# Rows for the first two expert tiles gathered from a copy of x in DRAM, with tokens found by one-hot products

## The chip, the cores and the metric

The kernel runs on one core of a Trainium2 chip. The metric is the device time of one execution in microseconds (us), the median over the runs shown. PE is TensorE, ACT is ScalarE, DVE is VectorE, POOL is GpSimd and SP is SyncE.

## What is computed

Three stages run in one program: causal-by-block attention (4 batches, 8 heads, 576 positions, head width 64), a mixture of 8 experts with hidden width 1024, of which each token takes one or none, and a dense two-layer network of hidden width 2048. The part around the change:

```python
x = attn_out.transpose(0, 2, 1, 3).reshape(2304, 512)
do_compute = (x @ w_skip) > 0            # the others pass through
logits = x[do_compute] @ w_gate
e_idx = argmax(logits, axis=1)           # one of 8 experts
gate_w = softmax(logits)[e_idx]
for e in range(8):
    h = relu(x[e_idx == e] @ w1[e])
    y[e_idx == e] = gate_w * (h @ w2[e])
x = x + y
# then: h = x @ w_in; out = (max(h,0) + alpha*min(h,0)) @ w_out
```

## The kernel before

**Attention** works on 16 pairs of heads (four pairs to a batch). SP's queue feeds it with one `load_step(n)` for each pair: it waits for `split_done` (POOL has split the queries and keys of the next pair into high and low parts), issues six loads of q and k for pair n+2 (lines 364 and 367), the two copies of `q_t` for the first head of pair n+1 (`swap`, line 388, which waits for ACT's evacuations `qk_evac`), three loads of v, the other two copies, and 512 KB of zeros into `x_slots`. In pairs 1 to 8 the queue also issues 1 MB of expert weights in each pair (lines 426 and 428). All of SP's DMAs go in one queue in this order. PE's first scores of pair n+1 wait for the first head's two copies (`swapped[0]`). The results for tokens land in `x_tok` (128 tokens of a tile on the partitions, 18 tiles, 512 columns), and the last 64 tokens of each batch first in `x_tail`, which ACT copies into the last two tiles of `x_tok` when attention is over.

**Routing** is a chain of small operations on DVE, with PE's products `RANKS` and `COUNTS` in the middle. It ends with `slot_i` (line 1192): for each token, the row of `x_slots` at which it is to stand, so that the tokens of an expert fill whole tiles of 128 rows. The semaphore `routed` goes out with it. POOL then issues 18 indirect DMAs (line 555), one for each tile of `x_tok`, which scatter the tokens' rows into `x_slots` in DRAM; SP meanwhile writes 15 tiles of zeros into the unused part of `y_slots` (line 454). When all 18 scatters have landed SP loads the rows of expert tile 0, and when these have landed those of tile 1 (`load_rows`).

**An expert tile** takes 128 rows: ACT copies them from `rows_in` to `rows`, PE transposes them (line 773), DVE takes them out as `rows_t`, PE multiplies by `w1` (line 786, 64 matmuls), ACT and DVE make `h_hi` and `h_lo`, and PE multiplies by `w2` in three products (line 800, 24 instructions to a tile). There are 13 such tiles here: expert 0 has tile 0, expert 1 tile 1, and expert 2 tiles 2 and 3. Each `w2` is needed as high and low parts. For experts 0 and 1 ACT and DVE make them (lines 966 and 1229 the first halves, 972 and 1240 the second). From expert 2 on POOL makes the first halves (lines 575 and 578), and PE waits for them in `w2_split` ahead of line 800.

**POOL's order** is: the 18 scatters, a wait for both row loads (`rows_loaded`, line 559), two chunks of `w_in` of 1 MB each (`stage`, loaded at line 564 and split at 566 and 568, with one buffer for both), the first halves of `w2` for experts 2 to 7, and then the gathers and splits of the dense network.

## Time and profile before

| | |
|---|---|
| time, median of 3 runs | 910.12 us (907.75 to 910.98) |
| time of the profiled execution | 910.3 us |
| span from first to last instruction | 908.4 us |
| PE busy | 822.5 us, 91% of the span |
| DVE / ACT / POOL busy | 435.7 / 265.2 / 238.0 us |
| mean granted TensorE clock | 0.960 of full speed |

The profiled execution is within 0.2 us of the median, and 1.9 us of it lie outside the span. Attention ends at about 246 us, routing at 256.5 us, the first matmul of an expert tile starts at 288.95 us, and the dense network's first matmul at 484.77 us. Times in the rows below are microseconds from the start of the span.

### The profile page before, as it was taken

How to read it: one execution, taken by the hardware profiler on the slowest of the kernel's cores; microseconds unless marked ns; L12 is line 12 of the kernel's file. 1: busy time of each engine (PE TensorE's matmuls, PEld its weight loads, DVE VectorE, ACT ScalarE, POOL GpSimd, SP SyncE). 2: the span in 40 equal slices, each digit the busy share in tenths (PEclk: the TensorE clock that was granted, in tenths of full speed). 3: DMA queues.
4: the chain of work that ended last, by engine and by line, in shares of the span. 5: the costliest groups of instructions: out<-in, count | busy, mean ns of one | idle time of the engine just before them, and what ended most of it. 6: DMA issues, size and time to landing. Idle time of an engine off the chain costs nothing.

```text
span 908.4 us, 15588 instructions
## 1 busy us (share of the span) xinstructions
PE 822.5 (91%) x5243; PEld 724.0 (80%) x5244; DVE 435.7 (48%) x894; ACT 265.2 (29%) x643; POOL 238.0 (26%) x193
## 2 busy tenths in 40 slices
PE   6799999999703989999968999999999999999997
PEld 5588888888503979999857988998998998898986
DVE  3476776777741333323364554444354344443442
ACT  4466656656321212212311112112112112112111
POOL 6224244432053681230547861001001001000000
PEclk9899999999955999999997999999999999999999
DMA  6388888574166846613834312002002002000001
GB/s 127 75 237 211 228 230 207 145 174 112 37 228 236 301 185 208 229 48 127 311 141 116 91 35 70 0 0 69 0 0 69 0 0 69 0 0 35 1 1 35
DMA packets 95972, 99.66 MB, mean 110 GB/s; under 512 B 64336, under 2 KB 64336, under 8 KB 95440
## 3 DMA queue, kind: packets, MB, share of 16 engines
q1 hardware_dynamic: 87136, 70.79, 27.3%
q0 software_dynamic: 4448, 15.73, 5.5%
q10 hardware_dynamic: 4368, 12.88, 3.9%
q8 instruction: 11, 0.18, 0.1%
q14 instruction: 9, 0.07, 0.0%
HBM read 64.78 MB, written 24.12 MB: 98 GB/s over the span
## 4 chain that ended last, share of the span: by engine, by line
PE 75%; SPq 6%; POOL 5%; DMA 5%; issue 4%; DVE 3%; ACT 2%; DVEq 0%; ACTq 0%; POOLq 0%
PE bank L836 22%; PE bank L847 22%; PE bank L786 7%; PE bank L800 7%; PE bank L685 4%; PE bank L696 3%; PE bank L673 3%; POOL x_slots L555 2%; PE bank L719 2%; PE bank L649 2%; SPq L364 2%; PE bank L667 1%; SPq L388 1%; DMA stage<-in_moe_w_in_dram 1%; POOL wi_lo L568 1%
## 5 line engine op out<-in xcount | busy, mean ns | idle before, releaser
L1287 DVE TENSOR_SCALAR g_sb<-bank,alpha_sb 128x384 f32<-128x384 f32 x96 | 59.3, 618 | 218.8 <-PE bank L836 218.6
L1005 ACT CAST g_hi<-g_sb 128x384 fp32r<-128x384 f32 x96 | 49.4, 515 | 322.0 <-DVE g_sb L1289 322.0
L836 PE MATMUL bank<-u_hi,wi_hi 128*128 128x384 f32 x384 | 130.5, 340 | 1.4 <-DVE u_lo L1260 1.4
L836 PE MATMUL bank<-u_hi,wi_lo 128*128 128x384 f32 x384 | 130.4, 340 | 0.0
L836 PE MATMUL bank<-u_lo,wi_hi 128*128 128x384 f32 x384 | 130.0, 339 | 0.0
L847 PE MATMUL bank<-wo_lo,g_hi 128*128 128x512 f32 x288 | 113.8, 395 | 0.0
L847 PE MATMUL bank<-wo_hi,g_hi 128*128 128x512 f32 x288 | 112.8, 392 | 0.8 <-DVE g_lo L1293 0.8
L847 PE MATMUL bank<-wo_hi,g_lo 128*128 128x512 f32 x288 | 113.5, 394 | 0.0
L786 PEld LDWEIGHTS bank<-rows_t,w_sb 128*128 128x128 f32 x832 | 96.5, 195 | 2.6 <-DVE rows_t L1208 1.5
L786 PE MATMUL bank<-rows_t,w_sb 128*128 128x128 f32 x832 | 96.8, 278 | 1.1 <-DVE rows_t L1208 1.1
L892 ACT ACTIVATE p_sb<-bank,neg_max 128x128 f32<-128x128 f32 (+2 forms) x144 | 79.2, 552 | 56.2 <-DVE neg_max L1034 53.7
L1034 DVE TENSOR_REDUCE neg_max<-bank 128x1 f32<-128x128 f32 (+2 forms) x144 | 72.7, 512 | 41.4 <-PE bank L675 20.0
L594 POOL DMA_INDIRECT u_sb<-y_slots,from_i x18 | 18.3, 1018 | 230.8 <-PE bank L824 214.5
L836 PEld LDWEIGHTS bank<-u_hi,wi_hi 128*128 128x128 f32 x384 | 73.1, 190 | 5.4 <-DVE u_lo L1260 1.8
L673 PE MATMUL bank<-k_t,q_t 128*128 128x128 f32 (+3 forms) x256 | 70.8, 371 | 7.2 <-DMA alpha_sb<-in_moe_alpha_dram 4.4
L836 PEld LDWEIGHTS bank<-u_lo,wi_hi 128*128 128x128 f32 x384 | 73.0, 190 | 3.6
L836 PEld LDWEIGHTS bank<-u_hi,wi_lo 128*128 128x128 f32 x384 | 72.9, 190 | 0.0
L685 PE MATMUL bank<-ident,p_sb 128*128 128x128 f32 x400 | 70.1, 287 | 1.8 <-DVE p_t L1048 0.4
L1048 DVE COPY p_t<-bank 128x128 f32<-128x128 f32 (+3 forms) x128 | 60.6, 484 | 17.2 <-PE bank L685 15.9
L523 POOL TENSOR_TENSOR parts<-qk_nat,zero_c 128x512 fp32r<-128x512 f32 (+1 forms) x28 | 31.5, 1148 | 124.8 <-DMA qk_nat<-in_k_dram 116.0
L847 PEld LDWEIGHTS bank<-wo_lo,g_hi 128*128 128x128 f32 x288 | 54.0, 188 | 11.7
L847 PEld LDWEIGHTS bank<-wo_hi,g_hi 128*128 128x128 f32 x288 | 54.1, 188 | 10.4 <-issue 1.4
(152 smaller groups left out, 1283.4 us busy)
## 6 DMA issues: line engine op xcount, KB each, us to landing
w_sb<-in_moe_w_dram ACTq DMA_DIRECT2D x6, 2048.0 KB, 7.8
w_sb<-in_moe_w_dram SPq DMA_DIRECT2D x6, 2048.0 KB, 8.7
q_t<-q_t SPq DMA_DIRECT2D x64, 160.0 KB, 2.5
w_sb<-in_moe_w_dram SPq DMA_DIRECT2D x16, 512.0 KB, 6.5
x_slots<-zeros SPq DMA_DIRECT2D x14, 512.0 KB, 3.6
v_nat<-in_v_dram SPq DMA_DIRECT2D x32, 128.0 KB, 2.4
y_out<-in_moe_w_out_dram POOLq DMA_DIRECT2D x16, 256.0 KB, 2.9
out_dram<-y_out SPq DMA_DIRECT2D x16, 256.0 KB, 2.7
```

The lines of the kernel that those rows point to most:

```text
L523: pool.tensor_tensor(to[:, lo:hi, 0:DH], nat[:, lo:hi], zero_c[:].unsqueeze(2).to_broadcast([P, hi - lo, DH]), ALU.add).then_inc(hi_done, 1)
L673: pe.matmul(a[:, 0:keys], q_t[:, par, z, h, P * (i + 1):P * (i + 2)], k_t[:, par, h, 0:keys], start=z == 0, stop=False)
L685: last = pe.transpose(t[:, P * j:P * j + P], p_sb[:, c % PB, P * j:P * j + P], ident[:])
L786: last = pe.matmul(HIDDEN[c][:, P * z:P * z + P], w1_sb[:, par, j, P * f:P * f + P], rows_t[:, j, :], start=j == 0, stop=j == KD - 1)
L800: last = pe.matmul(RESULT, h[:, f, :], w, start=f == 0 and z == 0, stop=f == KF - 1 and z == 2)
L836: last = pe.matmul(dst, w[:, j, P * f:P * f + P], u[:, j, :], start=z == 0, stop=z == len(terms) - 1)
L847: last = pe.matmul(YBANK[i][:, :], g[:, f % GB, P * i:P * i + P], w[:, f, :], start=f == 0 and z == 0, stop=f == FI - 1 and z == 2)
L892: act.activation(p_sb[:, c % PB, 0:keys], scores_ap(c), ACT.Exp, bias=neg_max[:, c:c + 1], accum_out=row_sum[:, par, i, h:h + 1]).then_inc ...
L1005: act.copy(g_hi[:, f % GB, :], g_sb[:, f % 2, :]).then_inc(g_hi_done, 1)
L1034: dve.reduce_max(neg_max[:, c:c + 1], scores_ap(c), AX.X, negate=True).then_inc(max_done, 1)
L1048: dve.tensor_copy(p_t[:, h, 0:i + 1, P * i:P * i + P], t[:, 0:P * (i + 1)].rearrange("p (j c) -> p j c", c=P)).then_inc(pt_evac, 1)
L1287: dve.tensor_scalar(g, a, 0.0, alpha_sb[:, f:f + 1], ALU.min, ALU.mult).then_inc(neg_done, 1)
```

## The change

Four things are done.

- **A copy of x.** SP writes `x_tok` and `x_tail` of each batch into a DRAM tensor `x_all` (`save_rows`): for batches 0 and 1 right behind the loops that load weights, for batch 2 behind `load_step(13)`, and for batch 3 in two parts at the end of attention. The weights are loaded in pairs 2 to 9 and no more in 1 to 8.
- **Tokens of the first two tiles.** DVE compares each token's slot with the rows and tiles (`at_row`, `at_tile`), and PE multiplies the one-hot matrices with the tokens' numbers (`NUMBERS`, 18 products of 4 columns; the numbers come from a product of constants, `COUNTING`, which ACT takes out); DVE turns the sum into `token_i`, the 128 token numbers of tile 0 and of tile 1.
- **Gathers.** POOL issues three scatters, then two indirect DMAs that gather the rows of tiles 0 and 1 from `x_all` straight into `rows_in`, then the other 15 scatters. It no longer waits for `rows_loaded`. SP no longer loads rows 0 and 1, and writes the zeros of `y_slots` only when both gathers have landed.
- **DVE's order.** `total` to `from_i` come behind `token_i`, and `rows_out(0)` comes between the two first-half subtractions of `w2`.

```diff
+    DIRECT = 2
+    AHEAD_OF_PICKS = 3
+            def save_rows(b, pairs):
+                lo, hi = P * pairs[0], P * pairs[1]
+                sp.wait_ge(x_done, 2 * (HP * b + pairs[1]))
+                sp.dma_start(x_all.rearrange("(t p) d -> p t d", p=P)[:, b * FULL:(b + 1) * FULL, lo:hi],
+                             x_tok[:, b * FULL:(b + 1) * FULL, lo:hi]).then_inc(x_saved, 16)
+                tail = B * MAIN + TAIL * b
+                sp.dma_start(x_all[tail:tail + TAIL, lo:hi], x_tail[:, b, lo:hi]).then_inc(x_saved, 16)
...
+            load_step(1)
             for par in range(2):
                 with sp.Fori(1, KD + 1) as m:
-                    load_step(m + KD * par)
+                    load_step(m + 1 + KD * par)
                     sp.dma_start(w1_sb[:, par, bass.ds(m - 1, 1), :],
...
+                save_rows(par, (0, HP))
-            with sp.Fori(2 * KD + 1, PAIRS - 2) as n:
+            with sp.Fori(2 * KD + 2, PAIRS - 2) as n:
                 load_step(n)
-            load_step(PAIRS - 2)
+            save_rows(2, (0, HP))
+            load_step(PAIRS - 2, False)
             sp.wait_ge(pv_done, 2 * (PAIRS - 1))
             load_v(PAIRS - 1)
+            save_rows(B - 1, (0, HP - 1))
+            save_rows(B - 1, (HP - 1, HP))
...
             used = sp.value_load(tile_hi[0:1, E - 1:E], min_val=1, max_val=MAX_TILES)
+            for g in range(DIRECT):
+                sp.wait_ge(rows_picked[g], 16)
+            sp.sem_inc(rows_loaded, 16 * DIRECT)
             with sp.Fori(used, SLOT_TILES) as g:
                 sp.dma_start(y_slots[bass.ds(g * P, P), :], zeros[:]).then_inc(y_zeroed, 16)
             sp.wait_ge(scattered, 16 * T_TILES)
-            sp.wait_ge(zeros_dma, ZEROED)
-            load_rows(0)
-            sp.wait_ge(rows_loaded, 16)
-            load_rows(1)
...
             for t in range(T_TILES):
+                if t == AHEAD_OF_PICKS:
+                    pool.wait_ge(x_saved, 16 * 2 * (B + 1))
+                    for g in range(DIRECT):
+                        pool.wait_ge(token_ready, 1)
+                        pool.indirect_dma_start(out=rows_in[:, g, :], out_offset=None, in_=x_all[:, :],
+                                                in_offset=bass.IndirectOffsetOnAxis(ap=token_i[:, g:g + 1], axis=0)
+                                                ).then_inc(rows_picked[g], 16)
...
-            pool.wait_ge(rows_loaded, 32)
...
+            for z, (lo, hi) in enumerate(PIECES):
+                pe.wait_ge(picks_ready, z + 1)
+                for t in range(lo, hi):
+                    last = pe.matmul(NUMBERS, at_row[:, t, :], id_at_tile[:, t].rearrange("p a g -> p (a g)"),
+                                     start=t == 0, stop=t == T_TILES - 1)
+            last.then_inc(tokens_done, 1)
...
             act.wait_ge(routed, 1)
-            rows_copy(0)
+            act.wait_ge(rows_picked[0], 16)
+            act.copy(rows[:], rows_in[:, 0, :]).then_inc(rows_copied, 1)
...
+            for lo, hi in PIECES:
+                part = [P, hi - lo, P]
+                dve.tensor_tensor(at_row[:, lo:hi], counting[:].unsqueeze(1).to_broadcast(part),
+                                  row_i[:, lo:hi].unsqueeze(2).to_broadcast(part), ALU.is_equal).then_inc(picks_ready, 1)
+            dve.wait_ge(tokens_done, 1)
+            step(dve.reduce_sum(token_f[:], NUMBERS.rearrange("p (a g) -> p g a", a=2), AX.X))
+            dve.tensor_copy(token_i[:], token_f[:]).then_inc(token_ready, 1)
...
-            for e in range(2):
+            first_lo(0)
             dve.sem_inc(y_evac, 1)
             dve.sem_inc(y_stored, 32)
             rows_out(0)
+            first_lo(1)
```

The first place is SP's queue at the end of the second loop that loads weights (`w_sb` are the weights, `qk_nat` the loads of q and k). Before:

```order
L428 DMA w_sb<-in_moe_w_dram 128x2x512
L424 REGISTER_ALU
L424 COMPARE_AND_BRANCH
L430 UNCONDITIONAL_BRANCH
L430 ISA
L364 ISA
L364 DMA qk_nat<-in_q_dram 128x4x64
L364 ISA
L364 DMA qk_nat<-in_q_dram 128x4x64
```

The same place in the changed kernel:

```order
L466 DMA w_sb<-in_moe_w_dram 128x2x512
L462 REGISTER_ALU
L462 COMPARE_AND_BRANCH
L435 DMA x_all<-x_tok 128x4x512
L438 DMA x_all<-x_tail 64x512
L469 UNCONDITIONAL_BRANCH
L469 ISA
L392 ISA
L392 DMA qk_nat<-in_q_dram 128x4x64
L392 ISA
L392 DMA qk_nat<-in_q_dram 128x4x64
```

Two writes to `x_all`, of 128x4x512 and 64x512 elements, now stand between the last weight load and the next loads of q.

The second place is POOL's instructions behind attention (`stage` is the buffer for `w_in`). Before:

```order
L555 DMA x_slots<-x_tok,slot_i 3584x512 x18
L564 DMA stage<-in_moe_w_in_dram 128x2048
L566 TENSOR_TENSOR wi_hi<-stage,zero_c 128x2048
L568 TENSOR_TENSOR wi_lo<-stage,wi_hi 128x2048
L564 DMA stage<-in_moe_w_in_dram 128x2048
```

Changed:

```order
L603 DMA x_slots<-x_tok,slot_i 3584x512 x3
L598 DMA rows_in<-x_all,token_i 128x512 x2
L603 DMA x_slots<-x_tok,slot_i 3584x512 x15
L611 DMA stage<-in_moe_w_in_dram 128x2048
L613 TENSOR_TENSOR wi_hi<-stage,zero_c 128x2048
L615 TENSOR_TENSOR wi_lo<-stage,wi_hi 128x2048
L611 DMA stage<-in_moe_w_in_dram 128x2048
```

Two gathers stand behind the third scatter, and 15 scatters come between them and the first load of `stage`.

The third place is DVE from `slot_i` to the subtraction of the second half of `w2` of expert 0 (`w_lo<-w_sb`). Before:

```order
L1192 CAST slot_i<-slot_f 128x18
L1195 TENSOR_REDUCE total<-excess 128x18
L1196 TENSOR_SCALAR total<-total 128x18
L1197 RECIPROCAL total<-total 128x18
L1198 TENSOR_TENSOR gate<-total,active 128x18
L1200 TENSOR_SCALAR tile_free<-hi_f 1x1
L1201 TENSOR_SCALAR from_f<-slot_f 128x18
L1202 TENSOR_TENSOR from_f<-from_f,active 128x18
L1203 TENSOR_SCALAR from_i<-from_f 128x18
L1229 TENSOR_TENSOR w_lo<-w_sb,w_hi_95 128x2048
L1229 TENSOR_TENSOR w_lo<-w_sb,w_hi_96 128x2048
L1208 COPY rows_t<-bank 128x512
```

Changed, from `slot_i` on, and then from `from_f` on:

```order
L1253 CAST slot_i<-slot_f 128x18
L1256 TENSOR_SCALAR row_i<-slot_i 128x18
L1257 TENSOR_SCALAR slot_tile_i<-slot_i 128x18
L1259 TENSOR_TENSOR at_tile<-counting,slot_tile_i 128x36
L1262 TENSOR_TENSOR id_at_tile<-at_tile,ids 128x72
L1266 TENSOR_TENSOR at_row<-counting,row_i 128x768 x3
L1270 TENSOR_REDUCE token_f<-bank_4 128x2
L1271 CAST token_i<-token_f 128x2
L1274 TENSOR_REDUCE total<-excess 128x18
```

```order
L1280 TENSOR_SCALAR from_f<-slot_f 128x18
L1281 TENSOR_TENSOR from_f<-from_f,active 128x18
L1282 TENSOR_SCALAR from_i<-from_f 128x18
L1308 TENSOR_TENSOR w_lo<-w_sb,w_hi_96 128x2048
L1287 COPY rows_t<-bank 128x512
L1308 TENSOR_TENSOR w_lo<-w_sb,w_hi_97 128x2048
```

Seven operations that make the one-hot matrices and two that make `token_i` stand ahead of `total`, and the copy to `rows_t` has moved between the two subtractions of 128x2048.

## Rows read from the trace of the kernel before

**Rows 1.** The page's chain that ended last, shares by engine.

```profile
PE 75%; SPq 6%; POOL 5%; DMA 5%; issue 4%; DVE 3%; ACT 2%; DVEq 0%; ACTq 0%; POOLq 0%
```

**Rows 2.** Waits, 236 to 350 us: who waited, for whom, total, times, longest.

```profile
PE bank L773 <- ACT rows L949: 33.0, 1, 33.0
...
POOL stage L564 <- DMA rows_in<-x_slots: 7.5, 1, 7.5
...
PE bank L800 <- POOL w_lo L578: 3.8, 1, 3.8
```

**Rows 3.** Chain in order of time, 236 to 345 us: start, us, what.

```profile
280.32 2.89 DMA x_slots<-x_tok,slot_i
...
288.83 5.45 DMA stage<-in_moe_w_in_dram
...
302.97 7.14 DMA stage<-in_moe_w_in_dram
...
322.10 6.45 POOL w_lo L578
...
328.68 7.39 PE bank L800 x24
```

**Rows 4.** Timeline of POOL: start, us, instruction, idle before it.

```profile
256.76 1.15 POOL L555 DMA_INDIRECT x_slots<-x_tok,slot_i  x1 [45.77 <-DVE slot_i L1192]
258.21 0.97 POOL L555 DMA_INDIRECT x_slots<-x_tok,slot_i  x1 [0.31 <-issue]
259.49 1.88 POOL L555 DMA_INDIRECT x_slots<-x_tok,slot_i  x1 [0.30 <-issue]
261.68 1.90 POOL L555 DMA_INDIRECT x_slots<-x_tok,slot_i  x1 [0.30 <-issue]
...
332.52 4.58 POOL L578 TENSOR_TENSOR w_lo<-w_sb,w_hi 128x2048 fp32r<-128x2048 f32 x1
```

**Rows 5.** Timeline of DVE, the same stretch.

```profile
256.28 0.17 DVE L1192 CAST slot_i<-slot_f 128x18 uint32<-128x18 f32 x1
...
257.50 0.38 DVE L1201 TENSOR_SCALAR from_f<-slot_f 128x18 f32<-128x18 f32 x1
...
258.20 4.54 DVE L1229 TENSOR_TENSOR w_lo<-w_sb,w_hi 128x2048 fp32r<-128x2048 f32 x2
```

**Rows 6.** Timeline of PE, the same stretch.

```profile
288.95 9.11 PE L786 MATMUL bank<-rows_t,w_sb 128*128 128x128 f32 x64 [1.13 <-DVE rows_t L1208]
...
303.92 7.30 PE L786 MATMUL bank<-rows_t,w_sb 128*128 128x128 f32 x64
```

**Rows 7.** Timeline of SP's queue: zero writes to y_slots.

```profile
257.53 15.43 SPq L454 DMA_DIRECT2D y_slots<-zeros  x15
```

**Rows 8.** Timeline of SP's queue in `load_step(5)` and `load_step(10)`.

```profile
90.94 1.48 SPq L364 DMA_DIRECT2D qk_nat<-in_q_dram  x2
...
95.58 1.15 SPq L367 DMA_DIRECT2D qk_nat<-in_k_dram  x1
97.12 1.28 SPq L388 DMA_DIRECT2D q_t<-q_t  x2
...
175.95 0.65 SPq L367 DMA_DIRECT2D qk_nat<-in_k_dram  x1
180.21 1.29 SPq L388 DMA_DIRECT2D q_t<-q_t  x2
```

**Rows 9.** Chain in order of time, 134 to 143 us.

```profile
137.39 1.15 SPq L367
...
139.66 2.50 DMA q_t<-q_t
```

**Rows 10.** Windows: us, busy time by engine, PEclk, DMA share, GB/s.

```profile
91.00:92.00 1.00, 1.00 (x8) 0.50 (x6) 1.00 (x3) 0.50 (x2) 0.00 (x0) 1.00 0.58 152
92.00:96.00 4.00, 4.00 (x55) 3.65 (x51) 2.95 (x12) 3.12 (x9) 0.00 (x0) 1.00 1.02 298
...
264.00:282.00 18.00, 0.00 (x0) 0.00 (x0) 0.00 (x0) 0.00 (x0) 13.33 (x14) 0.50 0.98 356
```

More of the change, by code:

```diff
@@ L86, in __call__ @@
                 return t
+        x_all = nc.dram_tensor("x_all", (B * S, D), F32, kind="Internal").ap()
         START = (nc.sbuf_base + 63) // 64 * 64
@@ L181, in program @@
         y_sb = sb("y_sb", [P, 2, D], F32)
+        picks = Region(REST, REST + half)
+        at_row = picks("at_row", [P, T_TILES, P], BF16)
+        at_tile = picks("at_tile", [P, T_TILES, DIRECT], BF16)
+        id_at_tile = picks("id_at_tile", [P, T_TILES, 2, DIRECT], BF16)
         stage = sb("stage", [P, 1, FD], F32)
@@ L194, in program @@
         zeros_dma = sem("zeros_dma")
+        x_saved = sem("x_saved")
+        counting_done = sem("counting_done")
+        counting_ready = sem("counting_ready")
+        picks_ready = sem("picks_ready")
+        tokens_done = sem("tokens_done")
+        token_ready = sem("token_ready")
+        rows_picked = [sem(f"rows_picked{g}") for g in range(DIRECT)]
         y_zeroed = sem("y_zeroed")
@@ L307, in program @@
         COUNTS = bank[5][:, 0:E + 1]
+        COUNTING, NUMBERS = bank[3], bank[4][:, 0:2 * DIRECT]
+        PIECES = [(z * T_TILES // 3, (z + 1) * T_TILES // 3) for z in range(3)]
+        AHEAD_OF_PICKS = 3
         HIDDEN = [bank[0], bank[1], bank[2], bank[5]]
@@ L388, in swap, with load_step @@
                         sp.dma_start(dst.bitcast(F32), src.bitcast(F32)).then_inc(swapped[h], 16)
-            def load_step(n):
-                if not isinstance(n, int):
+            def load_step(n, more=True):
+                if more:
                     sp.wait_ge(split_done, n + 1)
@@ L755, in _ @@
             to_rows(PAIRS - 1)
+            pe.wait_ge(router_const, 4)
+            pe.matmul(COUNTING[:, 0:P], ones_b[:], before[:], start=True, stop=True)
+            pe.matmul(COUNTING[:, P:P + 1], before[:], ones_b[:, 0:1], start=True, stop=True).then_inc(counting_done, 1)
             pe.wait_ge(member_ready, 1)
-            pe.wait_ge(router_const, 4)
             flat = member_b[:].rearrange("p t e -> p (t e)")
@@ L935, in _ @@
             last.then_inc(logits_tails, 1)
+            act.wait_ge(counting_done, 1)
+            act.copy(counting[:], COUNTING[:, 0:P])
+            act.copy(ids[:, :, 1], COUNTING[:, P:P + 1].to_broadcast([P, T_TILES])).then_inc(counting_ready, 1)
             act.wait_ge(x_done, 2 * PAIRS)
@@ L1229, in _ @@
                 dve.tensor_tensor(lo, raw, hi.bitcast(F32), ALU.subtract).then_inc(w2_split, 1)
-            dve.wait_ge(routed, 1)
+            first_lo(0)
             dve.sem_inc(y_evac, 1)
```

20 lines of the change are left out of this document (19 added, 1 removed).

## The prediction

> **What bounds the kernel now.** I read the page's chain that ended last first. It lies on PE for 75% of the span [rows 1], so time is won or lost only where PE waits, or where PE's wait moves. Around the change PE waits twice: 33.0 us for the rows of expert tile 0, and 3.8 us ahead of tile 2's second product, for `w_lo` from POOL (line 578) [rows 2]. The waits by length suggest that the 33.0 us are the prize. The chain in order of time says otherwise [rows 3]. It runs from the last scatter (280.32 us) through POOL's load of `stage` (288.83), the second load (302.97) and `w_lo` (322.10 to 328.55) to PE at 328.68. PE is not in it from 280 us to 328.68: tiles 0 and 1 run beside it. So the quantity to forecast is when POOL ends `w_lo` of expert 2. Tile 0 may start 20 us earlier, and PE only waits longer at tile 2 if POOL is not earlier too.
>
> On POOL, 18 scatters are issued from 256.76 us on; an undisturbed one takes 0.97 us, and 0.30 us pass to the next [rows 4]. The last starts at 280.32 [rows 3]: less what the first, third and fourth took too long (0.2 + 0.9 + 0.9), that is 1.265 us from one to the next. Then POOL waits 7.5 us for both row loads [rows 2], up to 288.83.
>
> In attention PE is full, and the link to watch is SP's queue. The end of a load of k (137.39 plus 1.15 us), then the copy of `q_t` (2.50 us from 139.66), lie in the chain [rows 9]: where SP is late with the loads, PE is late by as much. In `load_step(5)` SP ends its loads at 95.58 + 1.15 = 96.73 and issues the copies at 97.12, a margin of 0.39 us; in `load_step(10)`, without weights, the margin is 180.21 - 176.60 = 3.6 us [rows 8].
>
> **The change, part by part.** Sums are made against the profiled execution (910.3 us, of which 908.4 are the span), which is the median of 910.12 to within 0.2 us.
>
> *The writes to `x_all`, in attention.* One batch is 128x4x512 and 64x512 elements of 4 bytes, 1.18 MB. Those of batches 0 and 1 stand between the last weights and the next loads of q, where the margin is 0.39 us. There the DMA engines are full: share 1.02 from 92 to 96 us, with 0.58 in one microsecond ahead of it, 0.42 us of idle time to fill [rows 10]. At the 356 GB/s of the stretch that is full of 2 KB rows [rows 10] a batch takes 3.3 us. The loads and then the copies of `q_t` stand behind it in the same queue, so PE is late by 3.3 - 0.4 - 0.4 = 2.5 us, twice: 5.0 us. Bounds: only the two issues count, each like the 0.65 us of one small load [rows 8], 1.3 - 0.4 = 0.9 us each, 1.8 in all; or the mix runs at the 298 GB/s of 92 to 96 us [rows 10], 4.0 us each, 8 in all. Below nothing I see no reason: weights still go in 8 pairs, only one pair later. I take 5.0, since the trace shows full DMA engines and not just a busy queue. Batch 2 stands behind `load_step(13)` where no loads of q follow and the margin is 3.6 us: it costs nothing; with that cover gone it would be 2.5. Batch 3 goes out when attention ends, and has 10 us until POOL asks for it.
>
> *Routing up to `slot_i`.* `COUNTING` on PE, two copies on ACT and one multiplication on DVE lie in waits of their engines. `routed` becomes an instruction of its own: 0.1 us, so POOL starts at 256.9.
>
> *The tokens.* From 256.5 us DVE makes four small operations (0.2 each, 0.9 us together) and three compares of 768 columns. The subtraction of 2x2048 columns takes 4.54 us [rows 5], 1.11 ns a column, so 0.85 us each: they end at 260.0. Six products on PE that remain, and two small DVE operations, are some 1.4 us by the 0.17 us of `slot_i` [rows 5] and a guess of 0.1 to 0.15 us a product: `token_ready` at 261.4. Three scatters end at 256.9 + 3 x 1.265 + 0.2 = 260.9, plus a stretch, below: the gathers wait for almost nothing. I add 0.7 us, because a small DVE operation that started at 257.50, beside a scatter, took 0.38 instead of about 0.17 us [rows 5]: compares may be held up too.
>
> *The stretch of POOL's issues.* Two scatters took 1.88 and 1.90 us [rows 4], and both started inside DVE's subtractions of 258.20 to 262.74 [rows 5]: each ended about 0.9 us behind the end of the subtraction (260.47 and 262.74). So a scatter that starts in such an operation waits for its end. Before, that cost 0.92 + 0.94 us. Now five come among POOL's issues: the compares (once 0.9 us), the first-half subtraction of expert 0 at about 263.3 (a scatter starts 0.9 us into it: 1.35), that of expert 1 and the second half of expert 0 back to back at about 268 to 272 (1.6 and 1.0), and the second half of expert 1 when tile 0 ends at 268 + 15 = 283 [rows 6] (1.6). Together 6.4 us, against 1.9 before.
>
> *POOL's chain.* 256.9 + 0.2 + 20 issues x 1.265 + 6.4 + 0.7 = 289.5 us for the first `stage` load, against 288.83: the 7.5 us of waiting are gone, and two gathers and the stretch have taken their place. Loads: 5.45 and 7.14 us before [rows 3]. The first had the DMA engines nearly to itself. Now the zeros of `y_slots` (15 issues over 15.4 us, before from 257.53 on [rows 7]) start only at some 266 us, and the weights of expert 2 are asked for when the scatters have landed and tile 0 is stored, about 292 us, in the middle of that load. I take 7.14 for both, +1.7 us; bounds 5.45 and 8.5. The last link, `w_lo`, took 6.45 us; undisturbed it takes 4.58 [rows 4], and now no long DVE subtraction falls into it, since tile 2 is then waiting: -1.9 us. In all +0.7 + 1.7 - 1.9 = +0.5 us: tile 2's second product starts 0.5 us later, beyond what attention added. Bounds: -6.7 (rival 2) and +4.
>
> The Trainium skill, page "SBUF — State Buffer", section "SBUF: two separate sides", says that the port pair which VectorE and GpSimd share is an exclusive lock, held for the whole instruction, and that an operation with two SBUF inputs takes part. The stretched scatters agree. But the scatter from 258.21 ran in 0.97 us [rows 4] inside a subtraction that was not slowed either, which a strict lock excludes. What the strict lock would make of the time is rival 3.
>
> *Behind it.* Tile 0's first matmul comes at about 269 us (gather 262, landing 2.9 to 5.5 us later by rows of the same kind [rows 3], then 3.0 us for copy, transposes and copy), 20 us earlier. Tile 1 waits some 2 to 5 us for the rows of tile 2, which SP loads only behind the last scatter. Tile 2's first product ends near 308, and PE then waits some 20 us for `w_lo`. Late rows cost nothing until they eat these 20 us. After a long rest PE restarts slowly: in 264 to 282 us it is idle with a granted clock of 0.50 [rows 10], and the first 64 matmuls took 9.11 instead of 7.30 us [rows 6]. But before, the 24 matmuls behind `w_lo` took 7.39 us [rows 3], a slow start as well, so I add nothing (bound 1.8). From there everything is as before, on PE.
>
> **Sum:** 910.1 + 5.0 + 0.5 = 915.6 us.
>
> **The rivals.**
>
> 1. *The copies of x are hidden (not slower).* If PE's margin at the copies of `q_t` is wider than SP's, or the DMA engines take the 1.18 MB beside the rest, the 5.0 us vanish: 910.1 + 0.5 = 910.6 us. It decides once a batch makes the copies late by less than 0.4 us. For it speaks that load pairs with weights mostly keep PE's pace; against it, that with 1 MB the margin is already 0.39 us [rows 8] and once was gone [rows 9].
> 2. *POOL is not stretched.* Then 20 issues end at 282.4 and `stage` is asked for at 284.0 with the 1.6 us of compares and tokens, 4.8 us earlier than before, with loads as before: -4.8 - 1.9 = -6.7 us. 910.1 + 5.0 - 6.7 = 908.4 us. Against it stand the two rows of 1.9 us. Together with rival 1 it gives 903.4.
> 3. *A strict lock.* A long DVE operation then starts as a scatter ends and holds the next one, which comes 0.30 us later, for 2.27 - 0.3 = 2.0 us. Four of them cost 7.9 instead of 5.5 us, and `w_lo` ends 2.4 us later: 918.0 us. This is the skill's rule of the page above taken at its word.
> 4. *The change does not do what it says*: the gathers land so late that tile 0 gains nothing. By the 20 us of slack at tile 2 this changes nothing in the sum.
>
> **How the numbers follow.** Forecast 0.50, rival 1 0.17, rival 2 0.13, both together 0.06, rival 3 0.13, others 0.01. A measurement of this kernel tells about 0.5%, 4.5 us, from no change: 905.6 and 914.7. Below 905.6 lie rivals 1 and 2 together and the edge of rival 2: 0.10. Above 914.7 lie rival 3 and 7 in 10 of the forecast (its own range is 912.5 to 918.5, by the bounds 1.8 and 8 of the copies and those of the loads): 0.49. The rest is 0.41. The range 906 to 919 leaves out the double rival and the upper edge of rival 3 and of the copies, under 2 in 10.
>
> **What would show it.** Two waits of PE at line 673's counterpart for `q_t`, 2 to 3 us each, in the pairs after the two writes; attention's end 5 us later. Tile 0's first matmul 12 us or more behind the third scatter but 20 us nearer to `slot_i` than the 32.7 us of before. Scatters of 1.9 to 3 us at each long DVE subtraction. The first `stage` load 32 to 33 us behind the first scatter (before 32.1). A wait of PE of about 20 us ahead of tile 2's second product, released by POOL's `w_lo`. The prediction is wrong if the `q_t` waits are missing, if `stage` starts under 29 us behind the first scatter, or if PE's wait at tile 2 is short.

## The result, and the profile of the changed kernel

The changed kernel takes 926.27 us (median of 4 runs, 924.19 to 929.65), the kernel before, beside it, 910.01 us (median of 4, 907.75 to 910.98). The ratio is 1.0177, with a 95% interval of 1.0149 to 1.0204: slower by 16 us, where 5.6 us were forecast. The profiled execution took 928.32 us, 2 us above its own median, with a span of 926.3 us against 908.4: 17.9 us more. These fall into three parts, each read between two points that both traces have: up to `slot_i` 12.2 us, from there to tile 2's second product 3.9 us, and behind it 1.8 us.

**Up to `slot_i`.** Waits of PE in attention, from 27 to 250 us (total, times, longest); before, the same line of the view read 0.5 us in all:

```profile
PE bank L720 <- DMA q_t<-q_t: 9.9, 4, 4.2
```

Two of the four waits, 4.13 and 4.2 us, stand behind the copies of batches 0 and 1. The other two (1.1 us at 72 us and 0.4 us at 100 us) come ahead of any copy.

The queue of SP around the first copy of x (start, us, instruction):

```profile
104.51 0.38 SPq L435 DMA_DIRECT2D x_all<-x_tok  x1
104.93 0.52 SPq L438 DMA_DIRECT2D x_all<-x_tail  x1
105.83 2.54 SPq L392 DMA_DIRECT2D qk_nat<-in_q_dram  x2
108.55 3.09 SPq L395 DMA_DIRECT2D qk_nat<-in_q_dram  x1
...
113.40 1.31 SPq L395 DMA_DIRECT2D qk_nat<-in_k_dram  x1
115.10 1.30 SPq L416 DMA_DIRECT2D q_t<-q_t  x2
```

The copy itself is issued in 0.9 us. What stands behind it is held up: one small load of q (L395) occupies the queue for 3.09 us, where loads of the same size took 0.65 and 1.15 us [rows 8]. The loads end at 114.71 us, the copies of `q_t` go out at 115.10, and PE waits 4.13 us. Windows of the same stretch (us; busy time of PE, of its weight loads PEld, of DVE, ACT and POOL; then granted clock, DMA share, GB/s):

```profile
110.00:114.00 4.00, 3.91 (x30) 3.20 (x29) 2.41 (x6) 3.21 (x10) 0.00 (x0) 1.00 1.06 367
114.00:118.00 4.00, 0.36 (x4) 0.12 (x2) 0.82 (x2) 1.32 (x3) 1.07 (x2) 0.81 0.81 180
118.00:122.00 4.00, 3.52 (x16) 3.52 (x17) 0.98 (x2) 0.46 (x2) 3.92 (x3) 0.50 0.81 193
```

The third column from the end is the granted clock. PE rests from 114.4 to 118.5 us, and in the next window, when it has work again, its clock is granted at 0.50, the lower of its two levels (1.2 of 2.4 GHz). So each early copy costs its wait, and then a stretch at half clock. The same comes again at 177 us, behind the copy of batch 1; there the clock falls only about a microsecond after PE has resumed (1.00 from 180 to 181 us, 0.50 from 182 to 184). No wait for `q_t` or for the rows stands behind the copies of batches 2 and 3.

**From `slot_i` to tile 2.** DVE (start, us, instruction); `slot_i` stood at 256.28 before [rows 5]:

```profile
268.50 0.18 DVE L1253 CAST slot_i<-slot_f 128x18 uint32<-128x18 f32 x1
...
269.78 2.69 DVE L1266 TENSOR_TENSOR at_row<-counting,row_i 128x768 bf16<-128x768 bf16 x3
...
274.77 2.29 DVE L1308 TENSOR_TENSOR w_lo<-w_sb,w_hi 128x2048 fp32r<-128x2048 f32 x1
...
280.64 2.28 DVE L1308 TENSOR_TENSOR w_lo<-w_sb,w_hi 128x2048 fp32r<-128x2048 f32 x1
282.84 2.29 DVE L1321 TENSOR_TENSOR w_lo<-w_sb,w_hi 128x2048 fp32r<-128x2048 f32 x1
```

POOL beside it (idle time before, in brackets):

```profile
269.04 1.14 POOL L603 DMA_INDIRECT x_slots<-x_tok,slot_i  x1 [45.72 <-DVEq L1254]
...
274.10 0.97 POOL L598 DMA_INDIRECT rows_in<-x_all,token_i  x1 [0.79 <-DVE token_i L1271]
275.38 2.52 POOL L598 DMA_INDIRECT rows_in<-x_all,token_i  x1 [0.30 <-issue]
...
280.79 2.97 POOL L603 DMA_INDIRECT x_slots<-x_tok,slot_i  x1 [0.30 <-issue]
284.06 1.90 POOL L603 DMA_INDIRECT x_slots<-x_tok,slot_i  x1 [0.30 <-issue]
```

Each issue that starts inside one of DVE's long subtractions ends 0.83 to 0.84 us behind that subtraction's end (275.38 + 2.52 = 277.90 against 277.06; 283.76 against 282.92; 285.96 against 285.13), much as before. The five stretched issues took 1.10, 1.42, 2.52, 2.97 and 1.90 us, 5.1 us more than five undisturbed ones. PE (tile 0's first product):

```profile
281.12 10.26 PE L841 MATMUL bank<-rows_t,w_sb 128*128 128x128 f32 x64 [1.11 <-issue]
```

It starts 12.6 us behind `slot_i`, where it was 288.95 - 256.28 = 32.7 us [rows 5, 6]: the change does what it says, by 20 us. And the chain that ended last (start, us, what) has none of it, as before [rows 3]:

```profile
299.88 8.77 DMA stage<-in_moe_w_in_dram
308.72 3.82 POOL wi_hi L613
312.61 4.61 POOL wi_lo L615
317.51 8.85 DMA stage<-in_moe_w_in_dram
326.43 3.60 POOL wi_hi L613
330.10 6.43 POOL wi_lo L615
336.54 3.57 POOL w_hi L622
340.17 4.50 POOL w_lo L625
344.80 7.57 PE bank L855 x24
```

From the first scatter to the first stage load it is 30.84 us (before 32.07). The two loads take 8.77 and 8.85 us (before 5.45 and 7.14), the second `wi_lo` 6.43, and `w_lo` 4.50 (before 6.45). So: -1.2 + 3.3 + 1.7 + 1.8 (the second chunk's splits) - 1.9 + 0.2 (the first chunk's splits and small gaps) = 3.9 us. The waits of 236 to 360 us show where the 20 us went:

```profile
POOL wi_hi L613 <- DMA stage<-in_moe_w_in_dram: 16.6, 2, 8.3
...
PE bank L855 <- POOL w_lo L625: 14.6, 1, 14.6
...
ACT h_hi L1018 <- remote: 11.2, 1, 11.2
...
PE bank L855 <- DVE h_lo L1296: 6.1, 1, 6.1
```

PE waited 3.8 us for `w_lo` before [rows 2]; now 14.6, and 6.1 more in tile 0's own second product, behind a late relu (last section).

**Behind tile 2.** The last 1.8 us: expert 7's second weights took 10.07 us to load, not 8.4 us, and `w_lo` behind them 6.45 us, not 4.51. The third experiment below shows such a load (10.16 us) and such a `w_lo` (6.46 us) without any copy of x, in a kernel that is no slower than the one before, so this part is taken as scatter between runs.

### The profile page after: what moved, and what is told of

The parts are those of the page before. It is cut to its first block, busy times and chain, and to the rows that moved or that the text cites. A ratio compares the mean times of both kernels' runs of the same rounds, so it can differ in the third digit from the quotient of the medians.

```text
span 926.3 us, 15629 instructions
## 1 busy us (share of the span) xinstructions
PE 829.4 (90%) x5263; PEld 728.7 (79%) x5264; DVE 437.3 (47%) x904; ACT 265.5 (29%) x645; POOL 245.6 (27%) x195
## 4 chain that ended last, share of the span: by engine, by line
PE 73%; POOL 7%; DMA 6%; SPq 4%; issue 4%; DVE 3%; ACT 3%; ACTq 0%; DVEq 0%; POOLq 0%
PE bank L891 21%; PE bank L902 21%; PE bank L855 6%; PE bank L841 6%; PE bank L732 4%; PE bank L743 4%; PE bank L720 3%; POOL x_slots L603 2%; PE bank L766 2%; DMA stage<-in_moe_w_in_dram 2%; PE bank L696 2%; PE bank L714 2%; DMA q_t<-q_t 1%; ACT p_sb L947 1%; POOL wi_lo L615 1%
## 5 line engine op out<-in xcount | busy, mean ns | idle before, releaser
L841 PEld LDWEIGHTS bank<-rows_t,w_sb 128*128 128x128 f32 x832 | 98.7, 198 | 2.7 <-issue 1.5
L841 PE MATMUL bank<-rows_t,w_sb 128*128 128x128 f32 x832 | 98.8, 281 | 1.1 <-issue 1.1
L720 PE MATMUL bank<-k_t,q_t 128*128 128x128 f32 (+3 forms) x256 | 70.6, 369 | 16.9 <-DMA q_t<-q_t 11.7
L891 PEld LDWEIGHTS bank<-u_hi,wi_lo 128*128 128x128 f32 x384 | 72.4, 189 | 0.0
L855 PE MATMUL bank<-w_hi,h_hi 128*128 128x512 f32 x104 | 43.7, 421 | 22.0 <-POOL w_lo L625 15.9
```

What stands on the lines that cost most here:

```text
L720: pe.matmul(a[:, 0:keys], q_t[:, par, z, h, P * (i + 1):P * (i + 2)], k_t[:, par, h, 0:keys], start=z == 0, stop=False)
L841: last = pe.matmul(HIDDEN[c][:, P * z:P * z + P], w1_sb[:, par, j, P * f:P * f + P], rows_t[:, j, :], start=j == 0, stop=j == KD - 1)
L855: last = pe.matmul(RESULT, h[:, f, :], w, start=f == 0 and z == 0, stop=f == KF - 1 and z == 2)
L891: last = pe.matmul(dst, w[:, j, P * f:P * f + P], u[:, j, :], start=z == 0, stop=z == len(terms) - 1)
```

## The experiments

Ratios are to the kernel before, which ran beside each of the others (medians of 908.9 to 910.9 us). Experiments 1 to 4 ran side by side, and so did 5 to 8, 9 and 10, 11 and 12, and 13 and 14: within such a group times can be compared directly, from group to group it is better to compare ratios.

**1. The copies of x alone**, in the kernel before, and nobody reads them. The weights move one pair later, as in the change.

```diff
+            load_step(1)
             for par in range(2):
                 with sp.Fori(1, KD + 1) as m:
-                    load_step(m + KD * par)
+                    load_step(m + 1 + KD * par)
...
+                save_rows(par, (0, HP))
...
```

> The kernel before with the four copies of x to DRAM and the weights one pair later, and nothing else of the change: nobody reads the copy. Theory A (the copies of batches 0 and 1 stand between weights and the next loads of q and k, PE waits 4.2 us for q_t and then pays about 1.8 us at the lower clock, twice): 12 us over the kernel before, 922 us, with attention's end 12 us later. Theory B (the 12 us come from the one-hot code or from POOL's and ACT's new work in attention): within 2 us of the kernel before, 910 to 912 us. By the prediction on record, 5 us: 915 us.

Measured: 922.55 us, ratio 1.0131 [1.0094, 1.0169]. PE's wait in attention, and the windows (columns as above):

```profile
PE bank L690 <- DMA q_t<-q_t: 8.2, 3, 4.0
```

```profile
112.00:116.00 4.00, 0.37 (x4) 0.13 (x2) 0.83 (x2) 1.32 (x3) 1.18 (x2) 1.00 0.77 172
116.00:120.00 4.00, 3.63 (x19) 3.64 (x19) 0.98 (x2) 0.46 (x2) 3.83 (x3) 0.58 0.81 196
```

The copies alone carry some 12 of the 16 us (922.55 - 910.93 = 11.6), with nothing of the gather in the kernel.

**2. The changed kernel with the copies of batches 0 and 1 later**, behind `load_step(10)` and `load_step(11)`, where no weights are loaded. Loads of q still stand behind each of them: only batch 2's copy, behind `load_step(13)`, has none.

```diff
-                save_rows(par, (0, HP))
-            with sp.Fori(2 * KD + 2, PAIRS - 2) as n:
-                load_step(n)
+            load_step(2 * KD + 2)
+            save_rows(0, (0, HP))
+            load_step(2 * KD + 3)
+            save_rows(1, (0, HP))
+            load_step(2 * KD + 4)
+            load_step(2 * KD + 5)
             save_rows(2, (0, HP))
```

> The changed kernel with the copies of batches 0 and 1 moved behind load_step(10) and load_step(11), where no weights are loaded and SP has 3.6 us of margin; the copy of batch 2 stays. Theory A (they are dear only beside the weights): the 12 us of attention vanish but for 0 to 2 us, and the kernel takes 912 to 915 us. Rival C (a copy of 1.18 MB costs wherever it stands, since its DMA time of 3.3 us or more goes before the loads of q and k): 4 to 6 us remain for each, 920 to 926 us.

Measured: 914.75 us, ratio 1.0047 [1.0029, 1.0065]. PE's wait for `q_t` is 0.4 us as before. The first late copy is issued at 171.38 us, and behind it the queue shows (end of the loads: 178.10 + 0.65 = 178.75):

```profile
173.47 2.70 SPq L392 DMA_DIRECT2D qk_nat<-in_q_dram  x2
...
179.66 1.19 SPq L416 DMA_DIRECT2D q_t<-q_t  x2
```

Two loads of q are held for 2.70 us here too, where the same two took 0.99 us at 199.29 us, with no copy ahead of them. But of the 3.6 us between the last load and the copies of `q_t` [rows 8] 0.9 us are left, and PE does not wait. The same bytes cost nothing where the queue has slack for them; that loads of q stand behind them is not enough to make them dear.

**3. The weights' shift alone**, experiment 1 without the copies.

> The kernel before with the weights loaded in pairs 2 to 9 and no more in 1 to 8, and nothing else. Theory A: no difference, 909 to 911 us. Rival D (the later weights run into something in pair 9 that costs a part of the 12 us): 2 us or more over the kernel before.

Measured: 911.52 us, ratio 1.0011 [0.999, 1.0032]: nothing. It is also the base that experiment 1 is read against: 11.0 us for the copies, to within about 4 us by the two intervals (10.8 us in the traces, up to `slot_i`), of which PE's waits for `q_t` are 8.2 - 0.5 = 7.7 us. The other 3.3 us are in PE's own work. Groups of PE from 27 to 255 us (busy us, mean ns | idle before), first with the copies, then without:

```profile
L702 PE MATMUL bank<-ident,p_sb 128*128 128x128 f32 x375 | 65.9, 288 | 1.6 <-DVE p_t L1065 0.4
...
L736 PE MATMUL bank<-w_route,o_t 128*128 (+1 forms) x160 | 24.5, 305 | 0.3 <-ACT o_t L916 0.3
```

```profile
L686 PE MATMUL bank<-ident,p_sb 128*128 128x128 f32 x375 | 65.0, 285 | 1.6 <-DVE p_t L1049 0.4
...
L720 PE MATMUL bank<-w_route,o_t 128*128 (+1 forms) x160 | 22.6, 288 | 0.3 <-ACT o_t L900 0.3
```

As many matmuls take 0.9 and 1.9 us longer, and those of the scores (line 690, line 674 without the copies) 0.4 us, 3.2 us in all: these are the stretches at the lower clock behind the two waits.

**4. The changed kernel with the 15 zeroings of `y_slots` late**, issued by POOL behind its halves of expert 5.

```diff
-            with sp.Fori(used, SLOT_TILES) as g:
-                sp.dma_start(y_slots[bass.ds(g * P, P), :], zeros[:]).then_inc(y_zeroed, 16)
...
+                if e == 5:
+                    used = pool.value_load(tile_hi[0:1, E - 1:E], min_val=1, max_val=MAX_TILES)
+                    with pool.Fori(used, SLOT_TILES) as g:
+                        pool.dma_start(y_slots[bass.ds(g * P, P), :], zeros[:]).then_inc(y_zeroed, 16)
```

> The changed kernel with the zeros of y_slots issued by POOL behind the halves of w2 for expert 5, where POOL waits 45 us, and no more by SP beside the scatters. In the changed kernel the two stage loads took 8.8 us each (before 5.5 and 7.1), a relu of tile 0 on ACT came 11 us late, and w2 of expert 2 was asked for 15 us late. Theory E (these come from DMA engines kept full by the zeros, which now start 25 us later than before): stage loads of 5.5 and 7.1 us, no late relu, 4 to 6 us off the changed kernel, 919 to 921 us. Rival F (the loads are long for another reason, such as the weights of two experts beside them): loads stay at 8 to 9 us and the time within 2 us of the changed kernel, 924 to 928 us.

Measured: 925.53 us, ratio 1.0172 [1.0144, 1.02]. The chain in order of time:

```profile
297.12 9.62 DMA stage<-in_moe_w_in_dram
...
315.36 8.95 DMA stage<-in_moe_w_in_dram
```

The stage loads are as long as ever, and the time is rival F's: the zeros, the first of the two reasons that the prediction gave for 7.14 us, are not it. The late relu of theory E shrank from 11.2 to 3.2 us, without a gain in time.

**5. The changed kernel with POOL's order turned round**: its halves of `w2` of experts 2 and 3 come ahead of the two chunks of `w_in`.

```diff
+            w2_half(2)
+            w2_half(3)
             for t in range(LATE):
                 pool.dma_start(stage[:, 0, :], wi_v[t]).then_inc(wi_loaded, 16)
...
-            for e in range(2, E):
+            for e in range(4, E):
```

> The changed kernel with one edit: POOL makes its halves of the second weight matrices of experts 2 and 3 before it loads and splits the two chunks of w_in, so that PE at tile 2 no longer stands behind the two stage loads. Theory G (POOL's order is what keeps tile 0's 20 us from arriving): the 14.6 us wait of PE for w_lo at tile 2 goes. What ends last there is then the weight of expert 2 itself, whose load was issued at 308 us in the changed kernel because of a late relu, and is some 14 to 18 us earlier when that relu is on time; w_hi and w_lo take 3.8 + 4.6 us behind the load. Tile 2's second product then starts 8 to 14 us earlier: 926.3 - 8 to 14 = 912 to 918 us. Rival H (PE loses elsewhere what it gains, since the weight of expert 2, not the stage loads, ends last): PE waits at the same place for as long, released by a load or by halves that follow the load, and the time stays within 3 us of 926.

Measured: 918.07 us, ratio 1.0074 [1.0052, 1.0095]: by the ratios 9 us less than the changed kernel. Theory G was right in direction, but its mechanism gave less than it said: tile 2's second product starts 335.30 - 265.20 = 70.1 us behind `slot_i` instead of 76.3, which is 6.2 us and not 8 to 14. PE's wait for `w_lo` is 7.2 us, and the second weights of expert 2, whose load took 15.40 us, now end last.

**6. The same with the late copies.**

> The edit of the run before (POOL makes the halves of experts 2 and 3 ahead of the w_in chunks), and the copies of x of batches 0 and 1 moved behind the last loads of q. Theory G with the copies' 12 us taken out as well: 914.75 (measured with the late copies alone) minus the 8 to 14 us of tile 2: 901 to 907 us, below the 910.9 of the kernel before. Rival H: 914 to 916 us, no gain over the late copies alone. Tile 2's second product would start about 75 us behind slot_i under H, and 60 to 68 us under G.

The late copies stand where experiment 2 has them, with loads of q behind them, and not "behind the last loads of q" as the expectation says.

Measured: 906.44 us, ratio 0.995 [0.9936, 0.9965], in theory G's range. Tile 2's second product starts 69.6 us behind `slot_i`, just outside G's 60 to 68. The chain:

```profile
284.79 10.83 DMA x_slots<-x_tok,slot_i
299.11 14.83 DMA w_sb<-in_moe_w_dram
...
324.26 7.57 PE bank L861 x24
```

The next link is in view: the last scatter lands 10.83 us after its issue, where it took 2.89 [rows 3]. SP waits for it before it loads tile 2's rows and, behind them in the queue, asks for expert 2's second weights.

**7. The kernel before with POOL's order turned round**, the control.

> The kernel before, with POOL's order turned round in the same way and nothing else. There tile 0 starts 32.7 us behind slot_i and PE waits only 3.8 us for w_lo at tile 2. Theory G: at most those 3.8 us can be won, 906 to 909 us, so the order is worth little without the early tile 0. Rival I (the order alone is the gain, and the early tile 0 is not needed): as fast as the run with both edits, 907 us or less. Third possibility: the stage loads, now 16 us later, delay nothing before the last tiles, but make the chunk splits collide with DVE's later subtractions: 911 to 914 us.

Measured: 904.78 us, ratio 0.994 [0.9926, 0.9955]. PE's wait for `w_lo` at tile 2 falls to 0.2 us. That explains 3.6 us of 5.7. In the traces tile 2's second product comes 3.4 us nearer to `slot_i` (69.0 against 72.4 us), and behind it nothing changes (579.5 against 579.7 us). The other 2 us have no cause that the trace shows; `slot_i` itself comes at 251.89 to 256.28 us in kernels whose attention is the same, which is scatter of more than that size. Rival I holds: with the new order the kernel without gathered rows is as fast as the one with them (904.78 and 906.44 us, intervals that overlap). The order itself gives more with them, 8.8 us from experiment 2 to experiment 6 by the ratios against 5.7 here, but that only makes up what they had cost.

**8. Fewer bytes, as many issues**: experiment 1, with batches 0 and 1 writing one of four full tiles and the tail, 0.39 MB each instead of 1.18.

> The kernel before with the weights one pair later and the copies of x that nobody reads (which took 922.55 us), but the copies of batches 0 and 1 write only one of four tiles of full rows and the 64 rows of the tail: 0.39 MB instead of 1.18 MB, with as many issues at the same places in SP's queue. Theory J (it is the bytes that make the queue late): 0.39 MB are 1.1 us at 356 GB/s, of which 0.4 us are margin, so PE waits about 1 us twice, stays near full clock, and the time is 911 to 914 us. Rival K (it is the issues behind a copy that are held, whatever their size: 3.1 to 3.4 us for a small load): PE still waits about 4 us twice and the time stays at 920 to 923 us.

Measured: 913.82 us, ratio 1.0043 [1.0023, 1.0062]. The waits, and the window behind the wait of 1.68 us:

```profile
PE bank L691 <- DMA q_t<-q_t: 3.8, 3, 1.8
```

```profile
115.00:119.00 4.00, 3.84 (x31) 3.38 (x31) 2.13 (x8) 0.46 (x2) 3.68 (x3) 1.00 0.83 207
```

The time is theory J's, and rival K's 4 us do not come: with a third of the bytes the small load of q behind the first copy took 0.92 us, with all of them 3.00. And this window has its clock at 1.00: a rest of 1.7 us was free of the restart that a rest of 4 us brought. But PE waits 1.7 and 1.8 us, not 1. The queue from the last load of weights to the copies of `q_t`, first with 0.39 MB, then with 1.18 MB (experiment 1):

```profile
102.66 0.77 SPq L442 DMA_DIRECT2D w_sb<-in_moe_w_dram  x1
...
111.82 1.30 SPq L391 DMA_DIRECT2D q_t<-q_t  x2
```

```profile
101.56 0.76 SPq L441 DMA_DIRECT2D w_sb<-in_moe_w_dram  x1
...
112.99 1.30 SPq L391 DMA_DIRECT2D q_t<-q_t  x2
```

Without a copy (experiment 3) it is 7.24 us from one to the other, with 0.39 MB 9.16, with 1.18 MB 11.43; behind the second batch 7.46, 9.33 and 11.37. So 0.79 MB more cost 2.3 and 2.0 us, which is 346 and 385 GB/s, and an estimated 0.8 us of each copy is left over that does not go by the bytes: 9.16 - 7.24 less 0.39 MB at that rate.

**9. Late copies, POOL's order and late zeros together.**

> The kernel with both edits (late copies of batches 0 and 1, POOL's halves of experts 2 and 3 ahead of the w_in chunks; 906.44 us) and a third: the 15 zeroings of y_slots are issued by POOL behind its halves of expert 5 instead of by SP at 267 to 283 us, among the scatters. There the last scatter took 10.8 us to land (2.9 before), and the rows of tile 2 and the second weights of expert 2, behind it in SP's queue, came 20 us late for ACT. Theory L (the zeros in the DMA engines are what holds the last scatter): it lands in 3 to 5 us, expert 2's weights are asked for 6 to 8 us earlier and tile 2's second product starts 6 to 11 us earlier: 896 to 901 us. Rival M (it is the 2 MB of first weights that ACT asks for at 278 us, as tile 0 now ends among the scatters): the last scatter still takes 8 us or more, and the time is 903 to 907 us.

Measured: 903.24 us, ratio 0.9914 [0.9889, 0.9939]. The last scatter landed in 4.52 us, as theory L has it, but the time is that of rival M: tile 2 gained only 4 us (318.73 - 254.02 = 64.7 us behind the first scatter, where it was 324.26 - 255.22 = 69.0). The load of expert 2's second weights kept its length:

```profile
293.63 14.78 DMA w_sb<-in_moe_w_dram
```

**10. Its control**, the kernel before with POOL's order turned and the zeros late.

> The kernel before with POOL's halves of experts 2 and 3 first (904.78 us) and its zeroings of y_slots late in the same way: no copies of x, no rows by token. There the last scatter lands in 2.9 us already and the zeros end at 273 us, long before the last scatter, so under theory L there is nothing to win: 903 to 907 us. If the zeros also slow what runs beside them before 273 us (POOL's scatters), 900 to 903 us. The difference to the run with all three edits is what gathering by token is worth once POOL's order and the zeros are out of its way: 4 to 9 us under L, nothing under M.

Measured: 905.59 us, ratio 0.993 [0.9907, 0.9954]: the late zeros give nothing there. Experiment 9 is 2.4 us below it, less than the 4 to 9 us of theory L and within the two intervals: so far the gathered rows are worth nothing that is clear of the scatter.

**11. A fourth edit: the first weights of an expert asked for later.** ACT issues them behind its next half of `w_hi`, so that for experts 3, 5 and 7 they no longer load beside the second weights of the expert ahead.

```diff
+            second_hi(0, 0)
             with act.Fori(0, E // 2 - 1) as e2:
                 for par in range(2):
-                    second_hi(par, e2)
                     tiles(2 * e2 + par)
+                    second_hi(1 - par, e2 + par)
...
-            second_hi(0, E // 2 - 1)
```

> The kernel with all three edits (903.24 us) and a fourth: ACT asks for the first weights of the next expert only behind its second half of w_hi. For experts 3, 5 and 7 that half waits for the second weights of the expert ahead, so these 2 MB no longer load beside the other 2 MB. At tile 2 the second weights of expert 2, issued at 293.6 us, took 14.8 us with the first weights of expert 3 beside them from 295.5 us on, while PE waited 7.4 us for what follows. Theory N (the two loads share the DMA engines, and the one that PE waits for is the one that should go alone): the load takes 9 to 11 us, tile 2's second product starts 4 to 6 us earlier, and the time is 897 to 900 us. Rival O (the load takes long because of rows, y and scatters, not because of the other weights, or the weights that are now late make tile 3 wait): the load still takes 13 us or more or PE waits at tile 3's first product, and the time is 903 us or more.

Measured: 898.09 us, ratio 0.9885 [0.9863, 0.9907], the fastest here. The chain from the last scatter on:

```profile
285.36 4.25 DMA x_slots<-x_tok,slot_i
293.43 9.29 DMA w_sb<-in_moe_w_dram
...
313.06 5.87 PE bank L862 x24
```

The load fell from 14.78 to 9.29 us, PE's wait for `w_lo` from 7.2 us to 1.5, and tile 2's second product came 5.3 us nearer to the first scatter (313.06 - 253.69 = 59.4 us), all as theory N has it. In the time it shows less clearly: by the ratios 2.6 us against experiment 9, with intervals that overlap. The Trainium skill, page "DMA: Bandwidth & Descriptors", section "Issuing engines are not separate DMA queues", says that transfers started by different engines run on the same 16 DMA engines and interleave. By that, the trace agrees: ACT's 2 MB stretched SP's 2 MB by 5.5 us.

**12. Its control**, the kernel before with POOL's order and ACT's order turned.

> The kernel before with POOL's order turned (904.78 us) and the same edit of ACT's order. Without the early tile 0 the second weights of expert 2 took 8 to 10 us and little of it was waited for at tile 2. Theory N gives 902 to 905 us; if the late first weights cost anything, 905 to 908 us. Its difference to the run with all edits is what the rows by token are worth once POOL's order, the zeros and the loads are out of the way: about 5 us under N, of 20 us that tile 0 starts earlier.

Measured: 905.43 us, ratio 0.9959 [0.9944, 0.9974]. ACT's order gains nothing there. This control has its zeros early, which by experiment 10 makes no difference. Against it the gathered rows are worth 7.3 us, clear of the scatter, once POOL's order, the zeros and the weights are out of their way.

**13. A quarter of the first weights**, in the changed kernel with the late copies.

```diff
-                    act.dma_start(w1_sb[:, par], w1_v[bass.ds(2 * e2 + par + 2, 1)].rearrange("a p t f -> p (a t) f")
+                    act.dma_start(w1_sb[:, par, 0:KD // 4], w1_v[bass.ds(2 * e2 + par + 2, 1), :, 0:KD // 4].rearrange("a p t f -> p (a t) f")
```

> The changed kernel with the late copies (914.75 us, stage loads of 8.06 and 8.88 us), in which ACT's loads of the first weights of experts 2 to 7 fetch only a quarter, 0.5 MB instead of 2 MB (the rest of the matrix stays that of an earlier expert, so the output is not the reference's). Theory F (the stage loads are long because the weights of experts 2 and 3 are loaded beside them; the zeros were shown not to be it): both stage loads fall to 5.5 to 7 us, POOL ends w_lo of expert 2 some 3 to 5 us earlier, and the time is 909 to 912 us. Rival Q (they are long for what else is in the queues: the last scatters, rows and y, or the second weights alone): both still take 8 us or more and the time stays at 914 to 916 us.

Measured: 909.77 us, ratio 0.9986 [0.997, 1.0002]. The first stage load took 8.36 us (8.06 without the cut), the second 7.20 (8.88). The time is in theory F's range, but neither theory holds for both loads.

**14. ACT's order turned without POOL's**, on the late copies.

> The changed kernel with the late copies (914.75 us) and ACT's first weights asked for behind its second half of w_hi, as in the run that took 898.09 us, but with POOL's order left as it is: the two w_in chunks ahead of the halves of expert 2. If the stage loads are long because of the first weights beside them (theory F), those of expert 3 are out of the way of the second stage load, which falls to some 7 us, and the time is 911 to 914 us. Since POOL's 37 us for the two chunks still stand ahead of w_lo (theory G), it can't come below 909 us. Rival R (the order of the weights is the gain and POOL's order is not needed): 906 us or less.

Measured: 911.63 us, ratio 1.0014 [1.0, 1.0029]. Rival R falls: the order of the weights without POOL's brings 3 us. The chain:

```profile
286.31 8.11 DMA stage<-in_moe_w_in_dram
...
303.89 5.18 DMA stage<-in_moe_w_in_dram
```

The second stage load, with the first weights of expert 3 out of its way, takes 5.18 us, no longer than the first one of the kernel before (5.45 us [rows 3]). The first is not made shorter by late zeros (9.62 us), by smaller first weights (8.36) or by their order (8.11). In every kernel with POOL's old order and gathered rows it is issued right at the end of the last scatter's issue, while scatters still land (299.88 against 298.93 + 0.96); before, POOL first waited 7.5 us for the row loads [rows 2], and by then all scatters had landed. That they share the way is the explanation left over. It was not tried by itself.

## Why the prediction was wrong

The direction and the place were right, the size was not: 16.3 us instead of 5.6. In the profiled execution 12.2 us lie in attention, where 5.0 were forecast, 3.9 between `slot_i` and tile 2, where 0.5 were, and 1.8 behind it. By the prediction's own steps:

- **The copies of x: the step that failed.** The sum had "3.3 - 0.4 - 0.4 = 2.5 us, twice: 5.0 us". The stretch up to `slot_i` took 12.2 us more in the trace, and the copies alone cost 11.0 us (experiments 1 and 3), beyond even the upper bound of 4.0 us each. The mechanism was as written: the loads of q behind the copy in the same queue, `q_t` late, PE waiting, batches 2 and 3 free. The 3.3 us for the bytes were right as well: experiment 8 gives 346 and 385 GB/s for 0.79 MB of them, where 356 were taken. Three terms were mis-sized.
  - The two deductions of 0.4 us each. The "margin" of 0.39 us ahead of the copies of `q_t` [rows 8] is no slack: when the queue is 4 us late, the same 0.39 us lie there (114.71 to 115.10 us). What `load_step(10)` has beyond it (3.6 less 0.39 us) is slack, as experiment 2 shows. Nor is there room for the 0.4 us of idle DMA engines in the sum that the runs give, below.
  - A part of each copy that does not go by its bytes, some 0.8 us (estimated in experiment 8). The prediction priced the bytes, and as a bound the issues, but never both. The two issues of a copy and what lies between them take 0.9 us of the queue (104.51 to 105.45 us), which fits; that they are the cause was not tried. 3.3 + 0.8 = 4.1 us is the wait that was measured.
  - The restart of PE. In the part on tile 0 the prediction read that a rested PE starts slowly and costs 1.8 us; it did not ask the same of the waits that it had just forecast. The two together cost 3.3 us (experiment 3).
- **Rival 1, copies hidden:** fell by experiment 1.
- **Tokens and stretch:** POOL waited 0.79 us for the tokens (0.7 was added), the stretch was 5.1 us instead of 6.4, and the first stage load came 30.8 us behind the first scatter instead of 32 to 33. Rival 2 (no stretch) fell, and so did rival 3 (strict lock, a longer stretch). The scatter from 280.79 us ended at 283.76 inside the next subtraction, which kept its 2.29 us: the strict lock of rival 3 does not describe that row either.
- **Stage loads:** 7.14 us each were taken, 8.8 came, above the bound of 8.5. Of the two reasons given, the zeros play no part (experiment 4), and weights beside the load do, but those that ACT loads and beside the second load (5.18 us without them, experiment 14), where the prediction had SP's beside the first. Why the first is long stays open; that it shares the way with the last scatters was not tried.
- **`w_lo`, -1.9 us:** right to a tenth. But the collision with DVE had only moved: the second `wi_lo` took 6.43 us where the first took 4.61, with DVE's second-half subtraction beside it (from 328.78 us, 3.39 us instead of 2.29). The prediction took that subtraction out of one term and did not put it into the next.
- **PE's wait at tile 2, about 20 us:** 14.6 us there, and 6.1 us that PE had already waited in tile 0 for the late relu, which the prediction did not have. Tile 0 is 20 us nearer to `slot_i`, as forecast. Only the "12 us or more behind the third scatter" was off: 9.2 us.
- **Why 20 us at tile 0 gave nothing:** the reading from the chain was right and experiments 5 to 12 carry it further. Behind POOL's order stood the last scatter's landing, behind that the load of expert 2's weights. As each was removed, tile 2's second product came nearer to the first scatter: 75.8 us (changed kernel), 69.0 (experiment 6), 64.7 (9), 59.4 (11), where the kernel before has 71.9 [rows 3, 4].

## What to carry to other kernels

A transfer put ahead of loads in a queue costs its bytes and a fixed part, less the slack that the queue has at that place. A gap between two instructions is slack only if it shrinks when what stands ahead comes late: compare it in two traces before it is subtracted. A wait of PE that lets its clock fall has its restart added. When one stage is made to start earlier, walk the resources that the next stages need (a queue's order, an engine's order, a load's bandwidth) one after another: the gain arrives only when the last of them moves too. Here a new order of POOL's work in the kernel before gave 5.7 us for a few lines (experiment 7), and the gathered rows were worth 7.3 us only with the copies late and three such changes of order made (experiments 11 and 12).

## What was not expected of the hardware

- Each of the four rests of PE of 4.0 to 4.2 us (changed kernel and experiment 1) was followed by work at a granted clock of 0.50, for about 3 to 5 us; the rests of 1.7 and 1.8 us at the same places (experiment 8) were not (1.00). In one of the four the clock fell within the rest (0.50 from 117 us on, PE resumed at 118.5), in another only after PE had resumed at 180.6 us (0.50 from 182 us on).
- One small load's issue on SP lasted 2.6 to 3.4 us behind a copy of 1.18 MB, and 0.9 to 1.2 us behind 0.39 MB.
- ACT's fourth relu of tile 0 came 11.2 us late in the changed kernel, with its input ready and its engine idle, and the trace gives "remote" as the reason. It shows in the five kernels with gathered rows and POOL's old order (3.2 to 11.7 us at that relu in four of them, 5.2 and 8.3 us at the third and fourth in experiment 14) and in none of the four with POOL's new order. In four of the five the relu came 1.9 to 2.3 us behind the issue of the first stage load; with the zeros late (experiment 4) it came 6.6 us ahead of that issue. Since PE waited for POOL there anyway it moves no sum above, but it made the weights of experts 2 and 3 late. Its cause stays open.
